# Weight loads moved from SyncE to GpSimd, and rows split ahead of weights, in a mixture-of-experts stage

## What is computed

```python
N, D, E, F = (2304, 512, 8, 1024)
logits = x @ w_gate
noisy_logits = logits + np.log1p(np.exp(x @ w_noise)) * noise
top2 = np.argpartition(-noisy_logits, 2, axis=1)[:, :2]
# top2_w: softmax over the two, per token
for e in range(E):
    for k in range(2):
        mask = top2[:, k] == e
        h = np.maximum(x[mask] @ w1[e], 0.0)
        out[mask] += top2_w[mask, k, None] * (h @ w2[e])
```

## Time and profile before

| what | value |
|---|---|
| time, median of 3 runs | 1077.6 us (1073.67 to 1077.87) |
| the profiled execution's own time | 1076.64 us |
| its span | 1074.8 us |
| PE busy | 968.9 us, 90% |
| DVE busy | 492.4 us, 46% |
| ACT busy | 389.4 us, 36% |
| POOL busy | 208.8 us, 19% |
| DMA through SP's queue | 99.01 MB, 36.0% of 16 engines' span |
| mean granted clock of TensorE | 0.965 |

### The profile page before, as it was taken

One profiled execution on the slowest core, in us unless ns is written; L12 is line 12 of the kernel. 1 busy time (PEld: TensorE's weight loads), 2 busy tenths in 40 slices (PEclk: granted clock), 3 DMA queues, 4 the chain that ended last, 5 costly groups with the idle time before them and its releaser, 6 DMA issues.

```text
span 1074.8 us, 20634 instructions
## 1 busy us (share of the span) xinstructions
PE 968.9 (90%) x5392; PEld 820.4 (76%) x5393; DVE 492.4 (46%) x920; ACT 389.4 (36%) x649; POOL 208.8 (19%) x198
## 2 busy tenths in 40 slices
PE   9999999999999999999679999869466787999996
PEld 8889998989989989897558887647354565777885
DVE  4665533424334244466534444434545446454442
ACT  3247655555555555665011112212322223211111
POOL 4530000200202002004313222122111121322322
PEclk9999999999999999999989999989878888999999
DMA  9954610000000001431576675675566667567653
GB/s 303 302 162 136 231 53 1 3 29 1 30 0 0 29 0 66 151 147 41 146 180 137 141 137 119 160 177 122 158 177 176 191 140 188 120 144 140 143 111 80
DMA packets 290878, 128.11 MB, mean 119 GB/s; under 512 B 261885, under 2 KB 267389, under 8 KB 286720
## 3 DMA queue, kind: packets, MB, share of 16 engines
q1 hardware_dynamic: 268032, 99.01, 36.0%
q0 software_dynamic: 10992, 27.84, 8.8%
q10 hardware_dynamic: 11808, 0.68, 0.7%
HBM read 81.31 MB, written 20.37 MB: 95 GB/s over the span
## 4 chain that ended last, share of the span: by engine, by line
PE 64%; SPq 9%; issue 8%; DMA 5%; ACTq 4%; DVE 4%; ACT 3%; DVEq 2%; POOLq 0%; POOL 0%
PE bank L831 19%; PE bank L833 19%; PE bank L832 19%; SPq L541 3%; DMA h_there<-hid 3%; SPq L361 2%; SPq L534 2%; ACT ew L1263 2%; ACTq L361 2%; PE bank L781 2%; DMA raw<-w_ex 1%; PE bank L755 1%; ACTq L357 1%; DVEq L361 1%; PE bank L774 1%
## 5 line engine op out<-in xcount | busy, mean ns | idle before, releaser
L831 PE MATMUL bank<-ew,xgT_hi 128*128 (+1 forms) x328 | 136.2, 415 | 49.3 <-DVE xgT_lo L1658 44.5
L831 PE MATMUL bank<-ew,hT_hi 128*128 (+1 forms) x320 | 130.0, 406 | 41.6 <-DVE hT_lo L1664 41.6
L1242 ACT ACTIVATE hT_hi<-h_there 128x512 fp32r<-128x512 f32 x76 | 43.8, 624 | 283.9 <-DMA h_there<-hid 283.9
L832 PE MATMUL bank<-ew,xgT_hi 128*128 (+1 forms) x328 | 132.9, 405 | 0.0
L833 PE MATMUL bank<-ew,xgT_lo 128*128 (+1 forms) x328 | 132.7, 404 | 0.0
L831 PE MATMUL bank<-xs_hi,mw 128*128 128x384 f32 x384 | 129.9, 338 | 0.0
L833 PE MATMUL bank<-xs_hi,mw 128*128 128x384 f32 x384 | 129.5, 337 | 0.0
L832 PE MATMUL bank<-xs_lo,mw 128*128 128x384 f32 x384 | 128.9, 336 | 0.0
L833 PE MATMUL bank<-ew,hT_lo 128*128 (+1 forms) x320 | 127.7, 399 | 0.0
L832 PE MATMUL bank<-ew,hT_hi 128*128 (+1 forms) x320 | 127.6, 399 | 0.0
L831 PEld LDWEIGHTS bank<-ew,xgT_hi 128*128 128x128 f32 x328 | 64.9, 198 | 72.3 <-issue 59.1
(11 more groups left out here) (234 smaller groups left out, 1579.7 us busy)
## 6 DMA issues: line engine op xcount, KB each, us to landing
raw<-w_ex SPq DMA_DIRECT2D x32, 1024.0 KB, 5.0
h_there<-hid SPq DMA_DIRECT2D x156, 128.0 KB
x_there<-turned_x SPq DMA_DIRECT2D x152, 64.0 KB
stage<-w_ff SPq DMA_DIRECT2D x16, 512.0 KB, 3.3
out<-blank SPq DMA_DIRECT2D x3, 1536.0 KB, 11.0
x_rows<-x2sb SPq DMA_DIRECT2D x6, 768.0 KB, 3.8
kbuf<-kN SPq DMA_DIRECT2D x16, 256.0 KB, 4.4
vbuf<-vN SPq DMA_DIRECT2D x16, 256.0 KB, 5.1
```

The lines of the kernel that those rows point to most:

```text
L831: pe.matmul(o, a_hi, b_hi, start=first, stop=False)
L832: pe.matmul(o, a_hi, b_lo, start=False, stop=False)
L1242: nc.scalar.activation(h_hi[:, 4 * h:4 * h + 4, :], h_there[:, 4 * h:4 * h + 4, :], ACT.Relu).then_inc(hT_hi_done, 1)
```

## The change

The weight loads in the steps are issued by POOL, not by SP, on semaphores of their own (`ld_next`), and SP only moves. In POOL's step they stand between the gather of old rows and the scatter; ahead of the loop some stand before and some after the scatter of tile 1. On ACT and DVE the split of rows g+2 now stands ahead of the W1 quarter, and on DVE both turns of hidden g+1 stand behind it, so behind the rows too.

```diff
+        ld_next = [[sem(f"ld_next{p}{q}") for q in range(2)] for p in range(2)]
...
         def load_weights(eng, g, p):
             for q in range(2):
...
                     eng.wait_ge(w_lo_done[p], e * 2 + q + 3)
-                    load_raw(eng, expert, p, q)
+                    load_raw(eng, expert, p, q, ld_next[p][q])
...
@@ sync, ahead of the loop
-            sp.wait_ge(tab2_done, 1)
-            alone(sp, got_x[1], 32)
-            load_weights(sp, 0, 0)
-            load_weights(sp, 1, 0)
             sp.wait_ge(x2_stored, 16 * NCH)
...
             move_hidden(2)
             move_x(4)
-            load_weights(sp, 0, 1)
-            load_weights(sp, 2, 0)
-            load_weights(sp, 1, 1)
...
@@ sync, step
                     move_x(g + 3)
-                for of, p in (g + 1, 0), (g, 1):
-                    with sp.If(entry2(sp, T_BUSY, of, 0, 1)):
-                        load_weights(sp, of, p)
...
@@ gpsimd, step
-                gather_x(1 - s, i + s + 2, 2 * i + s + 2)
+                g = 2 * i + s
+                gather_x(1 - s, i + s + 2, g + 2)
                 old_rows(s, i + 1, (i + s) * 16)
-                send_rows(s, 2 * i + s + 1)
+                for of, p in (g + 1, 0), (g, 1):
+                    with pool.If(entry2(pool, T_BUSY, of, 0, 1)):
+                        load_weights(pool, of, p)
+                send_rows(s, g + 1)
...
@@ gpsimd, ahead of the loop
             gather_x(0, 3, 3)
+            pool.wait_ge(tab2_done, 1)
+            alone(pool, got_x[1], 32)
+            load_weights(pool, 0, 0)
+            load_weights(pool, 1, 0)
             send_rows(1, 2)
+            load_weights(pool, 0, 1)
+            load_weights(pool, 2, 0)
+            load_weights(pool, 1, 1)
...
@@ scalar, split_weights
-                            act.wait_ge(ld_raw[p][q], e * 16 + 32)
+                            act.wait_ge(ld_next[p][q], e * 16)
...
@@ scalar, step
+                split_moved_x(g + 2, s, g + 1)
                 split_weights(g + 1, 0)
-                split_moved_x(g + 2, s, g + 1)
                 split_weights(g, 1)
...
@@ vector, step
                 split_moved(g)
+                split_moved_x(g + 2, s)
+                split_weights(g + 1, 0)
                 turn_hidden(g + 1, 0)
-                split_weights(g + 1, 0)
                 turn_hidden(g + 1, 1)
-                split_moved_x(g + 2, s)
                 split_weights(g, 1)
```

More of the change, by code:

```diff
@@ L374, in load_meta, with load_raw @@
             eng.dma_start(dst[:, s, :], lists[bass.ds(row, P), :]).then_inc(done, 16)
-        def load_raw(eng, e, p, q):
+        def load_raw(eng, e, p, q, done):
             k = 2 * p + q
@@ L379, in load_raw @@
                           w_ex[bass.ds(e * 4 + k, 1), :, :].rearrange("o p n -> (o p) n")
-                          ).then_inc(ld_raw[p][q], 16)
+                          ).then_inc(done, 16)
         def load_weights(eng, g, p):
@@ L504, in _ @@
                 for q in range(2):
-                    load_raw(sp, first, p, q)
+                    load_raw(sp, first, p, q, ld_raw[p][q])
             sp.wait_ge(rec_sent, 16 * 2 * TJ * LEAD_CHUNKS)
@@ L516, in _ @@
                     sp.wait_ge(w_lo_done[p], q + 1)
-                    load_raw(sp, second, p, q)
+                    load_raw(sp, second, p, q, ld_raw[p][q])
                 if p == 0:
@@ L1255, in split_weights @@
                         with act.If(entry2(act, T_SPLIT[q], g, 0, 1)):
-                            e = entry(act, T_E, g, 0, E - 2)
+                            e = entry(act, T_E, g, 1, E - 2)
                             par = entry(act, T_PAR, g, 0, 1)
                             free = entry2(act, T_FIRST, g, 0, MAX_TILES)
-                            act.wait_ge(ld_raw[p][q], e * 16 + 32)
+                            act.wait_ge(ld_next[p][q], e * 16)
                             act.wait_ge(m2_done if p else m1_done, free)
```

## The result

| | before | after |
|---|---|---|
| time, median | 1076.8 us (4 runs, 1073.67 to 1077.87) | 1151.72 us (4 runs, 1146.84 to 1152.35) |
| ratio, 95% interval | | 1.069 (1.065 to 1.073) |
| span of the profiled execution | 1074.8 | 1150.4 |
| mean granted clock of TensorE | 0.965 | 0.938 |

The change costs 6.9%. Slower was forecast, but as 1103, and 1151.72 lies outside the range of 1068 to 1132.

What follows compares the result with a forecast made beforehand. The prediction took the kernel to be bound by a ring of splits, turns and moves among ACT, VectorE and SP in the stage of small experts. Front -9, stage +8, loads +24, steady tiles +3 made +26: 1103 us, range 1068 to 1132.

Steps and rivals of the forecast that it cites:

- The ring: Each step's cycle of splits, turns and moves between ACT, VectorE and SP: 17.9 with a first W1 quarter, 11.3 without W1.
- X: ACT's first split of the landed rows, put 9.0 us after t, the start of the second turn of hidden.
- the new order's stage: Stage of small experts, where 24 weight quarters are split: 290.5 us without the loads' price against 282.3 before, +8.
- SP's blocks: Table reads and loads ahead of SP's moves, 10.9 us lost in one step; they go once loads leave SP.
- TensorE's stall: Ahead of the loop, TensorE stands 10.96 us near 530 because SP moves hidden tile 2 late; it should go.
- The rival of rows in time: Rows land early enough that ACT is not held, so freeing SP decides: -44, 1033 us; chance 0.07.
- GpSimd as the bound: Rival: load issues on GpSimd take far over 1.0 us, so scatter and old rows fall behind: about 1120; chance 0.06.
- that loads cost nothing: Rival: loads fill gaps between moves in the stage of small experts: +2, 1079 us; chance 0.23.
- Loads beside moves: In the stage of small experts, 20 loads issued just before moves delay them 1.2 us each: +24 (0 to 61).
- Steady tiles: Some 18 tiles outside the stage of small experts go from TensorE's 11.0 to 11.1 us to 11.3: +3 (0 to 5).
- Front: Ahead of the loop, a free SP removes TensorE's 10.96 wait, but the next row gather comes late: -9 (4 to 11).
- full price of the loads: Rival: each load in the stage of small experts makes rows 3.05 us late: +68 in all, 1145 us; chance 0.12.

Runs made afterwards that it cites:

- e3: The changed kernel with GpSimd's loads cut to 128 of 2048 columns each (other columns keep old weights): 1094.95 us, 1.018 of the kernel before.
- e9: The changed kernel with the old order on ACT and VectorE and GpSimd's loads cut to 128 of 2048 columns: 1035.85 us, 0.964 of the kernel before.
- e11: The changed kernel with loads cut to 128 of 2048 columns and scatter and old-row gather cut to 16 of 128 rows: 1081.14 us, 1.005 of before.
- e4: The changed kernel with the scatter and the gather of old rows cut to 16 of 128 rows: 1130.26 us, 1.051 of the kernel before.
- e1: The changed kernel with the old order on ACT and VectorE, loads still on GpSimd: 1084.87 us, 1.008 of the kernel before.
- e2: The kernel before with only the new order on ACT and VectorE, loads still on SP: 1115.84 us, 1.038 of the kernel before.
- e6: The changed kernel with the old order on ACT and VectorE and GpSimd issuing each load one step later: 1069.26 us, 0.992 of the kernel before.
- e5: The changed kernel, new order kept, with GpSimd issuing each load one step later: 1121.74 us, 1.039 of the kernel before.
- e8: The changed kernel with ACT back in its old order, VectorE still in the new one: 1178.03 us, 1.091 of the kernel before.

## Why the prediction was wrong

**What held.** The ring: X is the pivot; the new order's stage without the loads' bytes was put at 290.5 (its terms add up to 290.2) and measures 292.4 (e3), the old one's with SP free at 247 and measures 251.9 (e9), the order's price at 43 and measures 40.5 to 43.1. Part of the first agreement is luck: 7.1 of the 292.4 are the scatter and the old rows (e11 has 285.3), for which the prediction had nothing, and its ring was 5 too long. SP's blocks, ACT's wait of 9.85 for a load and TensorE's stall are gone. The rival of rows in time is out, as is GpSimd as the bound; that loads cost nothing is out by e3.

**The step that failed first: "Loads beside moves", 1.2 each.** The term was mis-sized: 48.1 / 20 = 2.4, so +48 for +24. The reason given was that a row move 3 us after the hidden one meets only the tail of a load, and the rows contradict it. A load beside the hidden move delays SP's own four issues, 3.0 to 5.7, so the row move starts 2.7 later (t+6.5) and still meets the load's rest. The one row at hand, 3.05 late (3.1 by its own times, 724.85 - 713.43 - 8.3), was the better measure, and it came from a load on the same queue; on another queue such a load cost no less (3.4 to 3.8). The Trainium skill (DMA: Bandwidth & Descriptors, Issuing engines are not separate DMA queues) says that DMAs of all issuers run on the same 16 engines and interleave, and that a second issuer saves only the issue time. By it the sum took 61, and the trace has 48, four fifths of it. A mean DMA share of 0.60 was no argument against: from 676 to 679 us, in the step shown, the share is 0.99 and the engines move 326 GB/s, against 184 in the same part of e3's step, where the share is about 1 too.

**The step that failed second: "Steady tiles", +3.** Here a mechanism is missing, not only a size: the measured +19.0 is 1.0 for each of 19 steps (11.6 in the first eight, 7.4 in the last eleven). I moved the weight work and the turns, and left the sum where it was, though on VectorE it now follows the turn of rows with nothing in between. So scatter and old rows moved from behind the row move onto it, which costs 6 to 12 of the 19 (e11 against e3, e4 against the changed kernel; 0.7 in the tile shown). The ring was also 0.3 short (11.6 in e4 for 11.3), so TensorE's 11.1 covers less of it: the other 6 to 7.

**Front, -9: measured -4.7.** The stall went and the late gather came, as named. But with the old order and the same late gather the front gains 8.4 (e1). So most of what is missing comes from the new order: the turn of hidden now waits for those late rows, which the term did not count. The prediction had only asked when the rows come, and not what its own new order hangs on them.

**The sum** in the prediction's terms: -4.7 for -9; the stage 58.2 for 32, of it 10.1 for 8 by e3 and 48.1 for 24 by the loads; steady 19.0 for 3; and 3.1 behind the last t, for which there was no term. Of the 3.1, 2.7 stand in the last tile's 24 matmuls of W2: they take 8.7 us at a granted clock of 0.66, after TensorE had stood 4.88, where before they took 6.0 at 1.00, after 3.22. The rival "full price of the loads" gave 1145, near the time, but by other parts: its 61 is too much and its 4 for steady tiles too little.

**Where the gain went.** Freeing SP was to give 35 in the stage; e9 shows 30.4 (282.3 to 251.9) when the loads carry little. It lacks the loads' bytes as well as SP's blocks, and the kernel before with small loads was not run, so how much of the 30.4 is SP's alone is not shown. With whole loads e1 gives it back: SP issued them behind the row move, GpSimd issues them as the quarter comes free, beside the hidden move, for 45.5. The net is +15.1 in the old order (282.3 to 297.4), and +35.6 in the new (e2's 304.9 to 340.5). So in both orders the move of the issuer loses in the stage, and the new order adds 43.1 to e1's.

What stays open: no kernel kept the loads off all moves without making the experts of one tile wait. e6 has none of the 30.4 in its stage, and how much of it can be had is not known. Nor is it known why the steady steps with VectorE's new order lose 11.7 in one kernel (e3) and 19.0 in another.

## What to carry to other kernels

A blocked issuing queue may be what keeps large transfers apart from small urgent ones; before freeing it, look when the large one will then start and price it by the rows seen beside such a move, not by the mean share of the engines: here the one row at hand gave 61, the trust in idle gaps 24, and 48 was measured. When an engine's order is changed, list every instruction of its step with its new time, also those whose place in the list is the same, and follow the transfers that each of them releases. Where two engines make a split in turn, an order changed on one of them has a price of its own, and the prices don't add: beside GpSimd's loads the kernel lost 9.1% with the new order on VectorE alone, 3.6% with it on ACT alone, 6.9% with it on both and 0.8% with it on neither. The second of the two must not be put to wait for what the first makes last.

## What the runs showed of the hardware

A 1 MB load issued by GpSimd keeps it only 0.58 us and lands 5.9 us after the issue (the median of 20 in the stage; 5.0 for the 20 that SP issued there before), but it stretches another queue's four issues of small packets from 2.99 to 5.72 us, as the two timelines of that step show: the price appears on the engine that issues the moves. One of the four issues takes it all, mostly the third. In eight steps of the changed kernel with a load beside the hidden move it takes 3.5 to 3.8 us where e3 has 0.8 to 0.9; the first, second and fourth stay at 0.6 to 0.7. In a ninth step the load goes out 1 us later, and there it is the fourth, with 5.6. In the earlier trace rows, with the load on SP's own queue, it is the third too, with 3.44. Why one issue takes it all is not known.

One scatter took GpSimd three times as long as usual. The changed kernel's timeline ahead of the loop:

```profile
525.98 4.47 DVE L1694 TENSOR_TENSOR ew<-raw,ew 128x2048 fp32r<-128x2048 f32 x2
...
529.43 3.17 POOL L647 DMA_INDIRECT out<-ysb,meta_y  x1 [0.35 <-issue]
```

It takes 3.17 (3.14 before, in the same place) where the scatter of a steady tile takes 1.03, and its start lies inside VectorE's two weight rests, which end at 530.45. The other kernels agree: where this scatter starts 0.8 us or more before the rests end it takes 1.7 to 3.2, and where it starts later (e5 to e8) 1.07 to 1.19. No kernel changed this alone, so that the one causes the other is likely but not shown.
